# Attention of a fused attention and token-mixing kernel: pair parity on the rows of the scores, values in natural layout, scores read first

## What is computed

```python
B, H, S, D = 8, 8, 576, 64          # batches, heads, tokens, head size; chunk = 64
scores = scale * (q_c @ k_c.T)      # per batch, head and chunk: 64x64
attn = exp(scores - max) ; attn = attn / (sum(attn) + 1e-09)
x = attn @ v_c                      # then laid out as x[batch, token, 512]
# stage 2, per batch
h = relu(x.T @ w_tok1) @ w_tok2     # over tokens, 576 -> 256 -> 576
u = x + h.T
x2 = u + relu(u @ w_ch1) @ w_ch2    # over channels, 512 -> 1536 -> 512
# stage 3, per batch
a = relu(x2 @ w_in); u3, v3 = two halves of a
out = (u3 * (w_spatial @ normalised(v3) + b)) @ w_out
```

## Time and profile before

| | |
|---|---|
| Median of 3 runs | 1295.87 us (1295.0 to 1297.81) |
| The profiled execution: its time, its span | 1297.36 us, 1295.6 us |
| Granted TensorE clock, mean | 0.989 |
| TensorE matmul busy | 1263.4 us, 98% |
| VectorE, ScalarE, GpSimd busy | 508.9 us (39%), 349.4 us (27%), 101.9 us (8%) |
| DMA | 70.30 MB, mean 54 GB/s |

### The profile page before, as it was taken

One profiled execution on the slowest core, in us unless ns is written; L12 is line 12 of the kernel. 1 busy time (PEld: TensorE's weight loads), 2 busy tenths in 40 slices (PEclk: granted clock), 3 DMA queues, 4 the chain that ended last, 5 costly groups with the idle time before them and its releaser, 6 DMA issues.

```text
span 1295.6 us, 20569 instructions
## 1 busy us (share of the span) xinstructions
PE 1263.4 (98%) x8571; PEld 1082.2 (84%) x8571; DVE 508.9 (39%) x1044; ACT 349.4 (27%) x682; POOL 101.9 (8%) x73
## 2 busy tenths in 40 slices
PE   6899999999999999999999999999999999999998
PEld 5677887887887887887887888888998998998997
DVE  4344234234234334334334222125562562563451
ACT  4432122122122122122122111122432432432332
POOL 0550100100100100100100122104000000000000
PEclk7899999999999999999999999999999999999999
DMA  8623123123123113213210031120211111031002
GB/s 206 183 40 62 23 60 62 22 61 63 27 56 64 49 35 63 59 24 63 60 25 21 33 115 33 33 73 33 74 42 33 54 53 41 1 99 49 1 2 73
DMA packets 185069, 70.30 MB, mean 54 GB/s; under 512 B 161872, under 2 KB 171728, under 8 KB 184976
## 3 DMA queue, kind: packets, MB, share of 16 engines
q1 hardware_dynamic: 184976, 68.98, 20.8%
HBM read 50.05 MB, written 18.87 MB: 53 GB/s over the span
## 4 chain that ended last, share of the span: by engine, by line
PE 90%; DVE 6%; ACT 2%; issue 1%; SPq 1%; DMA 0%
PE acc L1178 21%; PE hid L1163 20%; PE acc L1038 15%; PE hid L1038 9%; PE side L1038 8%; PE side L1047 3%; PE side L1073 2%; PE side L1059 2%; PE side L1121 2%; PE side L1105 2%; PE side L1110 1%; PE side L1066 1%; PE side L1094 1%; DVE prob L826 1%; DVE prob L839 1%
## 5 line engine op out<-in xcount | busy, mean ns | idle before, releaser
L846 DVE SCALAR_TENSOR_TENSOR hidl<-hid,hidh 128x512 fp32r<-128x512 f32 x108 | 74.7, 692 | 279.9 <-ACT hidh L688 279.9
L1178 PE MATMUL acc<-hidh,w2h 128*128 128x512 f32 x432 | 174.2, 403 | 0.0
L1178 PE MATMUL acc<-hidh,w2l 128*128 128x512 f32 x432 | 169.3, 392 | 0.0
L1178 PE MATMUL acc<-hidl,w2h 128*128 128x512 f32 x432 | 169.3, 392 | 0.0
L688 ACT ACTIVATE hidh<-hid 128x512 fp32r<-128x512 f32 x108 | 64.3, 596 | 285.1 <-PE hid L1163 285.1
L1178 PEld LDWEIGHTS acc<-hidh,w2l 128*128 128x128 f32 x432 | 81.5, 189 | 17.7
L1163 PE MATMUL hid<-uh_a,w1h 128*128 128x512 f32 x240 | 96.1, 401 | 0.0
L1178 PEld LDWEIGHTS acc<-hidh,w2h 128*128 128x128 f32 x432 | 81.4, 188 | 16.9
L1178 PEld LDWEIGHTS acc<-hidl,w2h 128*128 128x128 f32 x432 | 81.5, 189 | 15.1
L1163 PE MATMUL hid<-uh_a,w1l 128*128 128x512 f32 x240 | 93.8, 391 | 0.0
L1163 PE MATMUL hid<-ul_a,w1h 128*128 128x512 f32 x240 | 93.6, 390 | 0.0
(11 more groups left out here) (293 smaller groups left out, 2710.1 us busy)
## 6 DMA issues: line engine op xcount, KB each, us to landing
x2l_raw<-x_scratch SPq DMA_DIRECT2D x32, 256.0 KB, 4.8
out<-out_tile SPq DMA_DIRECT2D x32, 256.0 KB, 2.0
vn<-in_v SPq DMA_DIRECT2D x126, 64.0 KB, 2.4
qn<-in_q SPq DMA_DIRECT2D x28, 256.0 KB, 3.3
kn<-in_k SPq DMA_DIRECT2D x448, 16.0 KB, 1.8
w1l_raw<-in_moe_w_ch SPq DMA_DIRECT2D x6, 512.0 KB, 5.4
w2l_raw<-in_moe_w_ch SPq DMA_DIRECT2D x6, 512.0 KB, 6.3
x_scratch<-x_a SPq DMA_DIRECT2D x2, 1024.0 KB, 4.8
```

The lines of the kernel that those rows point to most:

```text
L846: return nc.vector.scalar_tensor_tensor(lo, src, 0.0, hi.bitcast(F32), op0=ALU.max, op1=ALU.subtract)
L1178: last = nc.tensor.matmul(acc[:, c, :], w, x, start=(f == 0 and e == 0), stop=(f == KF - 1 and e == len(ops) - 1))
```

## The change

The scores' products are arranged so that the row half of the output is the parity of the pair of heads, and both chunks' keys lie side by side in a column block. A full tile's probabilities are then transposed as before, but come out with the chunk on the partitions, which is how the values lie in memory; so v is loaded by the one natural DMA. PV's products take chunk a from row half a and write to column half a. For a short tile the softmax works on 128 partitions and 256 columns instead of 64 and 512. The SC behind a PV waits until that PV is finished (`side_full`); ScalarE and VectorE read the scores first and the PV result after them; VectorE does the norm and `xl` at the start of the next group, ahead of `hidden`; what writes the banks next waits for `xl` (`part_lo`).

```diff
+    def scores_first(side):
+        return [job for job in side if job[0] == "SC"] + [job for job in side if job[0] != "SC"]
...
+            if kind == "SC" and beside(b, t - 1):
+                return part_lo, parts["PV", b, t - 1]
...
-            def load_v(b, t):
-                for h2 in range(2):
-                    for a in range(rows(t) // CHUNK):
...
-                load_v(b, t)
+                load_natural(v_nat(b, t), v_in, b, t, v_loaded)
...
-                act.wait_ge(side_full, number["SC", b, t + 1] if kind == "PV" and beside(b, t) else number[job])
+                if kind == "PV" and beside(b, t):
+                    act.wait_ge(shifted, tile_no(b, t + 1) + 1)
+                act.wait_ge(side_full, number[job])
...
                 for g, (kind, f) in enumerate(GROUPS):
+                    for job in scores_first(behind(j, g - 1) if g > 0 else []):
+                        if job[0] == "SC":
+                            softmax_norm(job[1], job[2])
+                        elif job[0] == "PV":
+                            side_job(job)
                     if kind == "up":
                         hidden(j, f)
                     if j == 0 and g == 1:
                         turn(1, 0)
-                    for job in behind(j, g - 1) if g > 0 else []:
-                        if job[0] == "SC":
-                            softmax_norm(job[1], job[2])
...
-                    if place_ > 0 and not (kind == "SC" and beside(b, t - 1)):
+                    if kind == "SC" and beside(b, t - 1):
+                        pe.wait_ge(side_full, number["PV", b, t - 1])
+                    elif place_ > 0:
                         pe.wait_ge(*emptied(in_bank[n][place_ - 1]))
...
-                    for g in range(PAIRS):
-                        for e in range(2):
-                            for a in range(n // CHUNK):
-                                r, s = slice(e * D, (e + 1) * D), slice(a * CHUNK, (a + 1) * CHUNK)
-                                last = nc.tensor.matmul(two[s, e, g * CHUNK:(g + 1) * CHUNK], qt[r, g, s], kt[r, g, s],
-                                                        start=True, stop=True)
+                    for gg in range(PAIRS // 2):
+                        for a in range(n // CHUNK):
+                            s = slice(a * CHUNK, (a + 1) * CHUNK)
+                            for e in range(2):
+                                for y in range(2):
+                                    r, to = slice(e * D, (e + 1) * D), gg * n + a * CHUNK
+                                    last = nc.tensor.matmul(two[y * CHUNK:(y + 1) * CHUNK, e, to:to + CHUNK],
+                                                            qt[r, 2 * gg + y, s], kt[r, 2 * gg + y, s],
+                                                            start=True, stop=True)
...
-                                r, s = slice(e * CHUNK, (e + 1) * CHUNK), slice(a * CHUNK, (a + 1) * CHUNK)
-                                last = nc.tensor.matmul(two[s, e, 256 + g * D:256 + (g + 1) * D], pt[r, g, s],
-                                                        vt[r, g, a, :], start=True, stop=True)
+                    for h in range(H):
+                        y, blk, to = h // 2 % 2, h % 2 * 2 + h // 4, h % (H // 2) * D
+                        for a in range(n // CHUNK):
+                            r = slice(a * CHUNK, (a + 1) * CHUNK)
+                            last = nc.tensor.matmul(two[r, h // (H // 2), to:to + D],
+                                                    pt[r, blk, y * CHUNK:(y + 1) * CHUNK], vt[r, h * D:(h + 1) * D],
+                                                    start=True, stop=True)
```

More of the change, by code:

```diff
@@ L228, in build @@
         nat, at = {}, ring_at
-        for x in ("q", "k"):
+        for x in ("q", "k", "v"):
             nat[x], at = place(f"{x}_pro", [P, NT, H * D], F32, at)
-        v_pro, at = place("v_pro", [P, NT, PAIRS, 2, D], F32, at)
         q_t_odd, at = place("q_t_odd", [P, PAIRS, P], F32, at)
@@ L388, in prob_tile, with v_nat @@
         def prob_tile(b, t):
-            return prob[:, tile_no(b, t) % 2, :, :, :]
-        def v_tile(b, t):
-            return v_pro[:, t, :, :, :] if b == 0 else vn[:, later(b, t) % 2, :, :, :]
+            return prob[:, tile_no(b, t) % 2, :, 0:rows(t)]
+        def v_nat(b, t):
+            return nat["v"][:, t, :] if b == 0 else vn[:, later(b, t) % 2, :]
         def blocks(buf, b, t):
@@ L656, in side_job @@
                 elif kind == "PT":
[L657 removed]
+                    nc.scalar.copy(p_tile(b, t)[0:n, :, :], grouped[0:n, :, :]).then_inc(p_t_ready, 1)
                 elif kind == "PV":
                     dst = xh[:, t, :] if t < KS else x_rem[0:REM, :]
[L660 to L662 removed]
+                    nc.scalar.copy(dst.rearrange("p (z c) -> p z c", z=2), both(job)[0:n, :, VALUES]).then_inc(part_hi, 1)
                 elif kind == "M":
@@ L679, in exponentials @@
                 act.wait_ge(shifted, tile_no(b, t) + 1)
-                p = prob_tile(b, t)[0:rows(t), :, :, :]
+                p = prob_tile(b, t)
                 nc.scalar.activation(p, p, ACT.Exp, scale=SCALE).then_inc(exp_done, 1)
@@ L717, in _ @@
                             channel_high(CW_EARLY + f)
-                    for job in behind(j, g):
+                    for job in scores_first(behind(j, g)):
                         if job[0] == "SC":
@@ L920, in _ @@
                                 turn(1 + n // NT, n % NT)
-                        elif job[0] in TWO_PART:
+                        elif job[0] in TWO_PART and job[0] != "PV":
                             side_job(job)
@@ L1109, in side_job @@
                     for g in range(PAIRS):
-                        last = nc.tensor.transpose(bank[:, g * P:g * P + n],
-                                                   prob_tile(b, t)[0:n, g, :, :].rearrange("p e k -> p (e k)"),
-                                                   ident[0:n, 0:n])
+                        last = nc.tensor.transpose(bank[0:n, g * P:(g + 1) * P], prob_tile(b, t)[:, g, :], ident[:, :])
                 elif kind == "PV":
                     pe.wait_ge(p_t_ready, tile_no(b, t) + 1)
[L1115 to L1119, removed]
-                                r, s = slice(e * CHUNK, (e + 1) * CHUNK), slice(a * CHUNK, (a + 1) * CHUNK)
-                                last = nc.tensor.matmul(two[s, e, 256 + g * D:256 + (g + 1) * D], pt[r, g, s],
-                                                        vt[r, g, a, :], start=True, stop=True)
+                    pe.wait_ge((v_loaded if b > 0 else v_first)[t], max(b, 1) * DMA)
+                    two, pt, vt = both(job)[:, :, VALUES], p_tile(b, t), v_nat(b, t)
+                    for h in range(H):
[5 more added lines that the diff above has]
+                                                    start=True, stop=True)
                 elif kind == "M":
```

37 lines of the change are left out of this document (18 added, 19 removed).

## The result

The changed kernel takes 1302.5 us (median of 6 runs, 1302.2 to 1303.01) against 1295.44 us before (6 runs). The ratio is 1.0054, interval [1.0041, 1.0066]: 7 us slower. The profiled execution has a span of 1301.2 us, 5.6 more than before's.

What follows compares the result with a forecast made beforehand. TensorE, busy 98% of the span, was taken to bound the kernel. Terms -11.5 + 12.9 + 1.6 + 0.4 + 9.2 + 0 = +12.6 us, on the median 1295.87, gave 1308.5 us, range 1301 to 1316.

Steps and rivals of the forecast that it cites:

- the prologue's rival: Prologue: clock stays high, PV.1 to PV.3 cost half, TensorE's waits for `xl` shrink; 4 to 8 us, 1300 to 1304; 8%.
- PT's waits: In the blocks, PT's 14 waits of 0.8 us for the norm all go: -11.5 us.
- the short PT: PT.4, the short tile's transposes, moves 128 columns instead of 64, drain around them unchanged: +0.4 us.
- the prologue: Before the blocks: earlier loads and shorter softmax offset by PV on half the quarters: 0 us, between -4 and +3.
- PV of full tiles, +12.9: In the blocks, 28 full PVs use two quarters instead of four, 0.46 us more each: +12.9 us.
- The column rival: In PV, the limit is per column half, so diagonal products cost nothing extra: 1292.4 us, faster by 0.3%; 10%.
- the rival of one product at a time: PV's products run singly, with two row halves in one bank: 1.84 us per PV, 1334 us total; 7%.
- Short PV, +3.2: PV.4 of the short tile goes from two quarters to one, 0.46 us more, seven times: +3.2 us.
- short SC, -1.6: SC.4 of the short tile goes from two quarters to four, 0.23 us less, seven times: -1.6 us.
- SC's wait, +9.2: In the blocks, SC waits for PV's last matmul to finish, 28 times 0.33 us: +9.2 us, between 7.0 and 11.8.
- PT still waits: In the blocks, exp comes late and `xl` gates PT, so some or all of 11.5 us stays: 1312 to 1320; 8%.

Runs made afterwards that it cites:

- Kernel 3: The kernel before with only SC's wait for the PV ahead of it added on TensorE: 1306.56 us, ratio 1.0078.
- kernel 1: The kernel before with only the scores-first order of ScalarE and VectorE and the later bank release, old layout and DMAs: 1281.58 us, ratio 0.9885.
- kernel 5: The changed kernel with v in four DMAs per full tile and two for the short one: 1302.86 us.
- kernels 5 and 2: The 2 is the changed kernel with the old reading order of ScalarE and VectorE and the earlier bank release: 1317.4 us, ratio 1.0169 to before.

## Why the prediction was right

It said slower with 88%, 1308.5 us in 1301 to 1316; measured was 1302.5. That is inside the stated range, but under the forecast's own 1304 to 1314, in the stretch that was there for the prologue's rival. The mechanism in the blocks was right nearly to the term. Of the sizes, PT's waits were off by 1.8 us, the short PT by 1.2 and the prologue by 3.2, all three on the same side; they make up the 6 us between the sum of +12.6 and the table's +6.6.

- **PV of full tiles, +12.9.** From start to start of PV's first and last matmul it is 0.930 us instead of 0.477: 28 x 0.453 = 12.7. Two quarters on the diagonal take two instructions per beat. The column rival (0.46 would have stayed) and the rival of one product at a time (1.84) both fall. The Trainium skill, "TensorEngine Tiling (Array Packing)", Restrictions and Gotchas, forbids different row tiles the same PSUM bank; here such pairs went side by side at the full beat, writing different halves of the partitions, so nothing was serialised.
- **Short PV, +3.2, and short SC, -1.6.** 0.930 to 1.390 from large matmul to large matmul, +3.2. Of PV.3 with SC.4, +0.570 is 0.453 of PV and 0.343 of the wait, so SC.4 gave -0.226, -1.6 in all. On one quarter, too, the load (0.13 us) lies beside the matmul before it: 16 loads of one quarter start within 0.87 us (1.00 less 0.13), one every 58 ns. A list item of the Trainium skill, "TensorE: Matmul & The Clock Gate", Part 3, has loads overlap only matmuls of another row group, though the paragraph ahead of it in the same Part also lets a load for the background weight buffer go ahead; this trace contradicts the "only". That the load costs no time of its own also shows in the transposes: those of PT.4 now load 64 columns and start 0.108 us apart, just like those of a full PT, which load 128, and TQ's, which load 128 and move 64, start 0.062 apart. Here the distance goes by the columns moved.
- **SC's wait, +9.2.** 0.333 from PV's last to SC's first matmul instead of 0.038, and 0.048 for filling the array: 0.333 less 0.038 plus 0.048 is 0.343, times 28 is 9.6. Kernel 3 has it by itself (0.362).
- **PT's waits, -11.5: mis-sized, -13.3 in the table, -14 in kernel 1.** I took the 0.82 us of the earlier trace rows as the loss. That is the idle time after the last large matmul had left the array; but behind it PT would have started one pitch (0.23) after its start, as it does now. Before, it was 309.63 less 308.43, the start of the last large matmul in this row:

```profile
308.43 0.39 PE L1178 MATMUL acc<-hidh,w2l 128*128 128x512 f32 x1
```

  1.20 instead of 0.23: 0.97 lost, 14 times, and 1.00 from large matmul to large matmul. The table's sum is 14 times that, less the 0.7 of the new wait in the first block. The idle time leaves out the overlap that was lost too.
- **Short PT, +0.4: the sign was wrong, -0.8.** I priced the moving columns and took the drain around it as unchanged. Operands of 64 rows came 0.32 us behind the last large matmul (319.98 to 320.30), and the next large matmul 0.15 behind the last of them; those of 128 rows come 0.23 behind, and the next large matmul 0.03 behind the last (in the rows above PT.4 has no idle mark, PV has one of 0.35). The form 128x64 between full ones needs no pause; 0.705 became 0.590.
- **Prologue, 0: mis-sized, -3.2.** PV.0 came 1.6 us earlier (16.89) where I had 2, and by another way than I had: with natural DMAs the issues take longer, k is issued 2.3 us earlier and not 5, and kernel 5 shows that the number of DMAs does not matter. The estimate for half the columns, 0.42, was met (0.43). What I missed is the clock behind it. PV.1 and PV.2 did run for the most part at the low level that I had charged. But PV.4 ran at the high one, so it takes 1.07 us to the next matmul's start, against 0.95 at the low level before: 0.1 more, and not 0.7. And the large matmuls of the token mixing between PV.3 and PV.4, 0.43 apart at 41 to 43 us before, are 0.23 apart now. From the first token matmul to PV.4 it was 7.73 us (35.66 to 43.39) and is 5.76 (34.30 to 40.06), which is 2.0 of the 3.2. The windows of 40 to 50 us, before and then now:

```profile
40.00:50.00 10.00, 8.39 (x66) 6.21 (x56) 2.67 (x4) 6.32 (x9) 9.53 (x5) 0.83 0.65 173
```

```profile
40.00:50.00 10.00, 8.39 (x57) 6.82 (x56) 2.33 (x4) 5.40 (x8) 9.43 (x4) 1.00 0.50 99
```

  How the 3.2 divide between loads, clock and softmax is open. Part of it is chance: three executions with the old loads and four-quarter PV had the first `up` at 58.31, 57.37 and 56.32 (before, kernels 1 and 3), three in the new layout at 55.13, 54.92 and 54.60 (changed, kernels 5 and 2), 2.4 less in the mean.

The rival "PT still waits" fell: with 0.9 us of margin `xl` was in time everywhere, and the one wait left is for the norm. The rival of a better prologue came true in part: the clock did rise, but TensorE's waits for `xl` did not shrink as it had them (5.2 us became 4.8). That, PT's waits and the short PT are why the time lies near the lower end of the range.

## What to carry to other kernels

- Small products on parts of the array cost the number of instructions over the number of quarters in use: before choosing a layout, count the quarters that consecutive products touch. Here the layout that saves DMAs uses half of them, and a wait for TensorE's own result comes on top; the saved DMAs were worth little.
- When a change has several parts, price them apart: here the order alone was worth 14 us, and keeping the old layout would have made the same edit a gain of 1.1%.
- A wait of a pipelined engine costs the start-to-start distance less the normal pitch, not the idle time in the list. And a limit removed in a chain of transfers shows the next one: look at what is late next before counting the gain.

## What was unexpected of the hardware

- TensorE waiting for its own semaphore: 0.22 to 0.24 us idle on the load side, 0.34 us in all on two quarters and 0.36 on four, 28 times with hardly a difference.
- TensorE does not start a list of 64x64 products strictly in order: with eight instructions per quarter in a row, the next quarter starts about three beats of 58 ns before this one is done (1.15 us for 16 products instead of 1.84).
- A transpose with 128 rows and 64 columns of operand among full matmuls is quicker around its edges than one with 64 rows: 0.590 against 0.705 us for four, though it moves twice the columns.
